# An attention and two-MLP kernel: where VectorE splits the weights, builds the keys of chunk 1 and takes the low part of x

## The chip, the cores and the metric

The program runs on one core of a Trainium2 chip. Its engines are TensorE (PE, with its weight loads as PEld), VectorE (DVE), ScalarE (ACT), GpSimd (POOL) and SyncE (SP), which issues most transfers. Each engine works through its own instructions in the order in which they are written and meets the others at semaphores. The metric is the device time of one execution in microseconds (us), lower is better.

## The reference

A linear attention with a decaying state over 4 sequences of 768 tokens and 8 heads of 48 features, and two MLPs (384 to 2048 to 384) over the 3072 tokens:

```python
for t in range(S):
    cur = np.einsum('bhd,bhe->bhde', u[None] * kt, vt)
    y[:, :, t] = np.einsum('bhd,bhde->bhe', rt, state + cur)
    state = w[None, :, :, None] * state + np.einsum('bhd,bhe->bhde', kt, vt)
...
h = x @ w_in                                        # first MLP
x = (np.maximum(h, 0) + alpha * np.minimum(h, 0)) @ w_out
h = x @ w_in2                                       # second MLP
out = (h * np.tanh(log(1 + exp(h)))) @ w_out2
```

## The kernel before

**Numbers.** Every matrix product of the MLPs is made of three products of split values: high part of the weights by high part of the data, low by high, high by low. So each weight block (128 hidden units of 16, a "slot": 768 columns) is read raw, copied to its high part on ACT (`split_hi`, L808) and subtracted to its low part (`split_lo`) on DVE (L684), or for the slots in `pool_slots` (0, 6, 10, 14 of the first MLP) on POOL (L461). Three raw buffers rotate: SP loads slot i when slot i - 3 has its low part.

**Attention.** The 3072 tokens are 24 chunks of 128; a chunk has two units v of two pairs of heads each. For a unit, keys (L315) and queries (L305) are scaled by powers of the decay, PE forms blocks of scores at seven levels (`score`, L1068, 104 small products), ACT writes the diagonal (`fill_diagonal`, L837) and copies the large blocks (`copy_high`, L849), DVE puts in the small ones with predicated copies, "the picks" (`pick_scores`, L601, 8 or 10 of them), and PE multiplies by the values and the state (`attend`, L1085 and L1091). `sum_state` (L1042) on PE and `advance_state` (L580) on DVE carry the state from chunk to chunk. When both units of a chunk are attended, ACT writes the high part of x (`x_hi_part`, L858 and L859), DVE the low part (`x_lo_part`, L617 and L619), and SP and ACT move rows of them between partitions (`fill_holes`, L325).

**Stages.** `first_tile` does attention alone, units 0 to 9 (chunks 0 to 4). PE scores unit v, in even v sums the state, multiplies the identity with itself (`warm`, L984, a result that nobody reads) and attends unit v - 1. DVE takes the picks of v and then scales keys (chunk c + 1) itself; POOL scales queries. `tile1` (t = 1 to 6) follows: 96 steps s, in each of which PE does `up(s)` (L1010, nine products of 128x512), then `down(s - 2)` (L1026, nine more), and between them in even steps `attend` of unit 8 + s/2 and `score` of unit 9 + s/2, in every fourth step (s = 3, 7, ...) `sum_state`. ACT takes both halves of the rectifier (L894, L895), DVE joins them (`activate`, L690), ACT writes the high part (`hi_part`, L814) and DVE the low part (`lo_part`, L674) of the result. `up(s)` waits for the low part of step s - 2, since two banks `hid` alternate. In even steps DVE then takes the picks of the unit scored in that step. In the tile t = 1 the splits of the first MLP's weights lie between: ACT in step j writes the high part of slot j + 4, DVE in step j the low part of slot j + 3. `tile2` is the second MLP, with no attention.

**The order around the change.** In the order on DVE all of it is written out by hand: activate, advance_state, x_lo_part, lo_part, picks, split_lo, sum_diagonal (L610). On ACT in an odd step: rectifier, hi_part, fill_diagonal of the coming unit, split_hi. On POOL two waits hold back work in chunk 5 until DVE's splits of slots 2 and 3 are done.

## Time and profile before

| | us |
|---|---|
| median of 3 runs | 991.45 |
| lowest and highest | 991.1, 991.75 |
| the profiled execution, its own time | 988.31 |
| its span, first to last instruction | 986.6 |
| busy in the span: PE, PEld | 964.5, 784.4 |
| DVE, ACT, POOL | 675.1, 618.9, 375.8 |

The profile has the program in 24025 instructions. PE is busy 98% of the span, and its granted clock has a mean of 0.992 of full speed (2.4 GHz). A time in a timeline is counted from the start of the span; "idle before <- X" names what ended an engine's idle time. The first matrix product of the first MLP starts at 62.97 us; before it lies the attention alone.

### The profile page before, as it was taken

To read this page: it belongs to the slowest core of one execution; us is meant where nothing else is said; L and a number is where in the kernel's file an instruction comes from. 1 tells how busy PE (TensorE), PEld (TensorE's weight loads), DVE (VectorE), ACT (ScalarE), POOL (GpSimd) and SP (SyncE) were. 2 spreads that over 40 slices of the span, in tenths; PEclk is the share of its full clock that TensorE was granted. 3 is DMA by queue.
4 is the path that set the end of the run, shared out by engine and by line. 5 is a ranking of instruction groups with operands and counts; after the bars stand their busy time and mean duration, and the time that the engine had idled before them with its cause. 6 is when DMAs were issued, how large, how long until landed. Compare 5 with 4: busy or idle time off the path is not lost.

```text
span 986.6 us, 24025 instructions
## 1 busy us (share of the span) xinstructions
PE 964.5 (98%) x9508; PEld 784.4 (80%) x9508; DVE 675.1 (68%) x1405; ACT 618.9 (63%) x1274; POOL 375.8 (38%) x664
## 2 busy tenths in 40 slices
PE   7889899999999999999999999999999999999997
PEld 4668678888888888888888888888888888888886
DVE  8997786666666666666653337877777777677775
ACT  6765545545554554455445658878777777787774
POOL 9989676667666676666501430000000000000000
PEclk8999899999999999999999999999999999999999
DMA  6353322111211131112004330000000000000000
GB/s 185 101 146 111 109 62 73 53 47 55 82 57 46 46 94 46 45 46 62 14 8 162 96 128 33 33 1 33 33 33 33 1 32 0 16 16 0 33 1 32
DMA packets 24617, 54.35 MB, mean 55 GB/s; under 512 B 4928, under 2 KB 12736, under 8 KB 24512
## 3 DMA queue, kind: packets, MB, share of 16 engines
q1 hardware_dynamic: 22688, 43.45, 14.8%
q10 hardware_dynamic: 1824, 9.47, 2.4%
q8 instruction: 70, 1.15, 0.5%
q14 instruction: 35, 0.29, 0.1%
HBM read 41.10 MB, written 9.44 MB: 51 GB/s over the span
## 4 chain that ended last, share of the span: by engine, by line
PE 89%; DVE 6%; ACT 2%; issue 1%; DMA 1%; SPq 0%; POOL 0%; DVEq 0%; ACTq 0%; POOLq 0%
PE acc L1026 40%; PE hid L1010 28%; PE lev L1010 10%; PE lev L1068 6%; DVE scores L601 3%; PE tok L1091 2%; PE tok L1085 2%; PE tok L1042 1%; DVE w_lo L684 1%; DVE hid L690 1%; DVE arena L315 1%; DMA neg_slope<-slope 1%; ACT scores L837 0%; PE hid L1068 0%; ACT w_hi L808 0%
## 5 line engine op out<-in xcount | busy, mean ns | idle before, releaser
L1010 PE MATMUL hid<-x_parts,w_hi 128*128 128x512 f32 x864 | 290.4, 390 | 0.6 <-DVE g_lo L674 0.6
L1026 PE MATMUL acc<-g_hi,w_hi 128*128 128x512 f32 x576 | 231.6, 402 | 0.0
L1026 PE MATMUL acc<-g_hi,w_lo 128*128 128x512 f32 x576 | 225.6, 392 | 0.0
L1010 PEld LDWEIGHTS hid<-x_parts,w_hi 128*128 128x128 f32 x864 | 162.6, 188 | 35.4 <-DVE g_lo L674 0.9
L601 DVE COPY_PREDICATED scores<-mask,lev 64x128 f32<-64x128 int8 x420 | 150.2, 358 | 29.9 <-ACT scores L849 18.1
L1010 PE MATMUL hid<-x_parts,w_lo 128*128 128x512 f32 x432 | 168.7, 390 | 0.0
L1026 PE MATMUL acc<-g_lo,w_hi 128*128 128x512 f32 x576 | 162.9, 391 | 0.0
L690 DVE SCALAR_TENSOR_TENSOR hid<-relu_neg,neg_slope,hid 128x512 f32<-128x512 f32 x96 | 72.5, 755 | 126.7 <-ACT hid L895 126.2
L894 ACT ACTIVATE relu_neg<-hid 128x512 f32<-128x512 f32 x96 | 57.3, 597 | 161.7 <-PE hid L1010 159.8
L1026 PEld LDWEIGHTS acc<-g_hi,w_hi 128*128 128x128 f32 x576 | 108.4, 188 | 23.9 <-issue 0.2
L1026 PEld LDWEIGHTS acc<-g_lo,w_hi 128*128 128x128 f32 x576 | 108.5, 188 | 23.2
L1026 PEld LDWEIGHTS acc<-g_hi,w_lo 128*128 128x128 f32 x576 | 108.6, 189 | 21.2
L305 POOL TENSOR_TENSOR arena<-arena,power 112x128 f32<-112x128 f32 x282 | 115.4, 444 | 2.1 <-DVE w_lo L684 2.1
L814 ACT ACTIVATE g_hi<-hid 128x512 fp32r<-128x512 f32 x96 | 57.5, 598 | 78.2 <-DVE hid L690 77.4
L455 POOL TENSOR_TENSOR arena<-arena,power_split 112x512 f32<-112x512 f32 x46 | 58.7, 1276 | 116.2 <-PE tok L1091 116.2
L737 DVE SCALAR_TENSOR_TENSOR arena<-arena 128x512 f32<-128x512 f32 x96 | 66.4, 692 | 51.7 <-ACT arena L934 51.7
L315 POOL TENSOR_TENSOR arena<-arena,power_rev 112x128 f32<-112x128 f32 x228 | 94.2, 448 | 19.2 <-PE lev L1068 17.6
L1010 PE MATMUL lev<-x_parts,w_hi 128*128 128x512 f32 x288 | 96.3, 389 | 0.0
L1010 PEld LDWEIGHTS hid<-x_parts,w_lo 128*128 128x128 f32 x432 | 81.4, 188 | 17.4 <-issue 0.2
L674 DVE TENSOR_TENSOR g_lo<-hid,g_hi 128x512 fp32r<-128x512 f32 x96 | 66.3, 691 | 39.5 <-ACT g_hi L814 39.3
L1068 PEld LDWEIGHTS lev<-arena 48*64 48x64 f32 x4472 | 74.3, 135 | 10.4 <-issue 10.4
L1068 PE MATMUL lev<-arena 48*64 48x32 f32 (+1 forms) x4472 | 79.1, 222 | 1.9 <-issue 1.2
(95 smaller groups left out, 1352.0 us busy)
## 6 DMA issues: line engine op xcount, KB each, us to landing
w_raw<-weights SPq DMA_DIRECT2D x32, 384.0 KB, 3.2
arena<-rkv SPq DMA_DIRECT2D x24, 384.0 KB, 3.2
arena<-rk_t SPq DMA_DIRECT2D x48, 192.0 KB, 3.4
arena<-rkv SPq DMA_DIRECT2D x24, 192.0 KB, 2.6
x_dram<-result ACTq DMA_DIRECT2D x6, 768.0 KB, 3.4
arena<-x_dram SPq DMA_DIRECT2D x6, 768.0 KB, 4.3
out<-result ACTq DMA_DIRECT2D x6, 768.0 KB, 3.3
x_parts<-y SPq DMA_DIRECT2D x142, 16.0 KB, 1.8
```

Of the source, the lines that this page charges most:

```text
L305: return engine.tensor_tensor(dst, src, spread(table[0:ROWS, pairs, 0:m], 2, CHUNK // (2 * m)), ALU.mult)
L315: return engine.tensor_tensor(dst, src, spread(table[0:ROWS, pairs, HALF - m:HALF], 2, CHUNK // (2 * m)), ALU.mult)
L455: nc.gpsimd.tensor_tensor(r_state[0:ROWS, x], spread(rk_rows[0:ROWS, par, 0, pairs], 1, 2), power_split[0:ROWS, :, pairs], ALU.mult).then_ ...
L601: nc.vector.copy_predicated(dst, pick, src).then_inc(pick_done if done < 2 * low_levels(rep) - 1 else mask_done, 1)
L674: nc.vector.tensor_tensor(g_lo[:, j % RING], hid[j % 2][:, 0:TILE], g_hi[:, j % RING].bitcast(F32), ALU.subtract).then_inc(glo_done, 1)
L690: nc.vector.scalar_tensor_tensor(hid[j % 2][:, 0:TILE], relu_neg[:, j % 2], neg_slope[:, j:j + 1], hid[j % 2][:, 0:TILE], ALU.mult, ALU.ad ...
L737: nc.vector.scalar_tensor_tensor(root[:, d], eps[:, d], 0.75, seed[:, d], ALU.add, ALU.mult).then_inc(root_done, 1)
L814: nc.scalar.activation(g_hi[:, j % RING], hid[j % 2][:, 0:TILE], ACT.Copy).then_inc(ghi_done, 1)
L894: nc.scalar.activation(relu_neg[:, j % 2], hid[j % 2][:, 0:TILE], ACT.Relu, scale=-1.0)
L1010: last = nc.tensor.matmul(to[:, 0:TILE], w[:, j, kt * P:(kt + 1) * P], x[:, par, kt], start=x is x_hi and w is w_hi and kt == 0, stop=x is ...
L1026: last = nc.tensor.matmul(acc[d][:, 0:TILE], w[:, j, cols], g[:, j % RING], start=j == 0 and g is g_hi and w is w_hi, stop=j == STEPS - 1 ...
L1068: last = nc.tensor.matmul(level_scores(banks, l)[tokens, 2 * q + u], k[rows, tokens], t[rows, wanted], start=True, stop=True)
```

## The change

It has five parts, none of which adds or removes work except three warm products on PE.

1. DVE in the tile t = 1: the splits of slots j + 3 are no longer done in each step behind the picks, but in step 0 (slot 3) and in odd steps (slots j + 3 and j + 4), where no picks are. sum_diagonal comes ahead of them.
2. ACT in the tile t = 1: in odd steps split_hi comes ahead of fill_diagonal, in even steps nothing changes.
3. DVE in the first stage: the keys of unit 2 (chunk 1) are scaled ahead of the first advance_state and picks; the low part of x for chunk 3 comes ahead of the picks of unit 8, not between the second and the third of them.
4. PE in the first stage: the warm products of unit 1 go (of 512 and of 256 columns); that of unit 9 and the last become three in a row.
5. PE: attend of unit 8 moves from the end of the first stage to step 0, behind up(0).

```diff
@@ attended_at
             v = FIRST - 2 + s // 2
-            return FIRST - 1 if s == 1 else v if s % 2 == 0 and FIRST <= v < UNITS else None
+            return FIRST - 2 + s if s < 2 else v if s % 2 == 0 and FIRST <= v < UNITS else None
@@ vector, first_tile
+                def keys_of(c, x):
+
+                    level = scale_half(c, x, False)
+                    for l in range(1, LEVELS):
+                        level(l)
...
+                    if v == 0:
+                        keys_of(1, 0)
                     if x == 0:
                         advance_state(c, token_bank(0, c))
                     if ends and x == 0:
-                        between = lambda n: x_lo_part(c - 1, 0, c - 1, token_bank(0, c - 1)) if n == 2 else None
-                    pick_scores(v, 0, between)
-                    if not ends:
-                        level = scale_half(c + 1, x, False)
-                        for l in range(1, LEVELS):
-                            level(l)
+                        x_lo_part(c - 1, 0, c - 1, token_bank(0, c - 1))
+                    pick_scores(v, 0)
+                    if not ends and v > 0:
+                        keys_of(c + 1, x)
@@ vector, tile1
                         pick_scores(unit, 1)
-                    if t == 1 and j < STEPS - EARLY and j + EARLY not in pool_slots:
-                        split_lo(j + EARLY)
                     if summing is not None and summing < CHUNKS - 1:
                         sum_diagonal(summing + 1, (summing + 1) % 2)
+                    if t == 1 and (j == 0 or j % 2):
+                        for i in range(j + EARLY, min(j + EARLY + 1 + j % 2, STEPS)):
+                            if i not in pool_slots:
+                                split_lo(i)
@@ scalar, tile1
                     hi_part(s, j)
+                    if unit is not None:
+                        copy_high(unit, 1)
+                    if t == 1 and j + EARLY + 1 < STEPS:
+                        split_hi(j + EARLY + 1)
                     if coming is not None:
                         fill_diagonal(coming)
-                    if unit is not None:
-                        copy_high(unit, 1)
                     if j == LAG1 - 1 and t > 1:
                         copy_out(t - 2, x2_dram[t - 2])
-                    if t == 1 and j + EARLY + 1 < STEPS:
-                        split_hi(j + EARLY + 1)
@@ tensor, first_tile
-                    for n in {0: (), 1: (PAIRS, PAIRS // 2)}.get(v, (PAIRS,)):
-                        warm(hid[1] if v == FIRST - 1 else acc[2], n)
-                    if v > 0:
+                    if PER_CHUNK <= v < FIRST - 1:
+                        warm(acc[2])
+                    if 0 < v < FIRST - 1:
                         attend(v - 1, 0)
-                warm(hid[1])
+                for _ in range(3):
+                    warm(hid[1])
```

How it moves instructions, at three places. First DVE in steps 2 to 4 of the tile t = 1 (g_lo is lo_part, scores the picks, w_lo a split, hid the activate). Before:

```order
L684 TENSOR_TENSOR w_lo<-w_raw,w_hi 128x768 [waits whi_done]
L690 SCALAR_TENSOR_TENSOR hid<-relu_neg,neg_slope,hid 128x512 [waits relu_done]
L576 MEMSET state 112x192 [waits av_done]
L674 TENSOR_TENSOR g_lo<-hid,g_hi 128x512 [waits ghi_done]
L610 TENSOR_REDUCE diag<-ruk 128x8 [waits fill_done,s_ruk]
L690 SCALAR_TENSOR_TENSOR hid<-relu_neg,neg_slope,hid 128x512 [waits relu_done]
```

The same stretch now, from the last of the picks of step 2 on:

```order
L601 COPY_PREDICATED scores<-mask,lev 64x4x2x16 [waits pick_done] x2
L692 SCALAR_TENSOR_TENSOR hid<-relu_neg,neg_slope,hid 128x512 [waits relu_done]
L576 MEMSET state 112x192 [waits av_done]
L676 TENSOR_TENSOR g_lo<-hid,g_hi 128x512 [waits ghi_done]
L608 TENSOR_REDUCE diag<-ruk 128x8 [waits fill_done,s_ruk]
L686 TENSOR_TENSOR w_lo<-w_raw,w_hi 128x768 [waits whi_done]
```

The split that stood between the picks of step 2 and activate of step 3 is gone from there, and one stands behind sum_diagonal of step 3.

Second, DVE at the start of the first stage, where the six rows of keys (arena<-arena,acc) of unit 2 move; a piece of the difference:

```order
-L601 COPY_PREDICATED scores<-mask,lev 64x4x8x4 [waits pick_done] x2
-L601 COPY_PREDICATED scores<-mask,lev 64x4x4x8 [waits pick_done] x2
-L315 TENSOR_TENSOR arena<-arena,acc 112x64x2 [waits score_done,rows_in1]
+L315 TENSOR_TENSOR arena<-arena,acc 112x64x2 [waits score_done,rows_in1,s_masks]
 L315 TENSOR_TENSOR arena<-arena,acc 112x32x4
 L315 TENSOR_TENSOR arena<-arena,acc 112x16x8
```

The keys stand now ahead of the first advance_state, and wait there for the scores of unit 0 and for the rows of chunk 1.

Third, PE between the scores of unit 9 (acc<-arena) and up(0) (hid<-x_parts). Before:

```order
L1068 MATMUL acc<-arena 64x32 x24
L984 MATMUL hid<-ident 128x512
L1085 MATMUL tok<-arena,state 48x128 x2
L1091 MATMUL tok<-scores,arena 48x128 x2
L1085 MATMUL tok<-arena,state 48x128 x2
L1091 MATMUL tok<-scores,arena 48x128 x2
L984 MATMUL hid<-ident 128x512
L1010 MATMUL hid<-x_parts,w_hi 128x512
```

Now:

```order
L1072 MATMUL acc<-arena 64x32 x24
L988 MATMUL hid<-ident 128x512 x3
L1014 MATMUL hid<-x_parts,w_hi 128x512
L1014 MATMUL hid<-x_parts,w_lo 128x512
L1014 MATMUL hid<-x_parts,w_hi 128x512
L1014 MATMUL hid<-x_parts,w_lo 128x512
L1014 MATMUL hid<-x_parts,w_hi 128x512
L1014 MATMUL hid<-x_parts,w_lo 128x512
```

attend of unit 8 (tok<-) no longer stands between the two warm products, but behind up(0).

## Rows read from the trace of the kernel before

**Rows 1.** Busy time by stretch: us, each engine's busy us, granted PE clock, DMA.

```profile
50.00:100.00 50.00, 46.56 (x751) 36.37 (x751) 40.70 (x91) 28.99 (x75) 46.05 (x76) 1.00 0.45 126
100.00:125.00 25.00, 21.86 (x298) 17.67 (x298) 19.27 (x42) 14.67 (x35) 15.34 (x27) 0.86 0.35 108
...
150.00:175.00 25.00, 25.00 (x338) 20.36 (x337) 16.63 (x39) 13.58 (x35) 17.05 (x35) 1.00 0.26 78
```

**Rows 2.** Waits of PE from 60 to 150 us: for whom, total us, times, longest.

```profile
PE tok L1091 <- DVE state L580: 2.2, 1, 2.2
...
PE tok L1042 <- DVE x_parts L619: 1.0, 1, 1.0
PE tok L1085 <- issue: 1.0, 1, 1.0
PE hid L1010 <- DVE g_lo L674: 0.6, 1, 0.6
```

**Rows 3.** The chain that ended last, behind the longest wait and later: start, us, what.

```profile
108.86 2.21 PE lev L1068 x86
111.07 4.14 PE acc L1026 x9
115.20 2.85 PE hid L1010 x9
...
122.15 0.57 PE tok L1091 x8
122.73 1.75 PE lev L1068 x94
124.48 2.28 PE acc L1026 x9
126.76 2.04 PE hid L1010 x9
```

**Rows 4.** Busy time in stretches of 2 us behind that wait, columns as in Rows 1.

```profile
110.00:112.00 2.00, 2.00 (x44) 1.76 (x37) 0.76 (x1) 1.18 (x3) 1.02 (x4) 0.50 0.09 28
...
116.00:118.00 2.00, 2.00 (x9) 1.59 (x8) 1.88 (x5) 0.00 (x0) 1.92 (x3) 0.81 0.00 0
```

**Rows 5.** Timeline of DVE in steps 3 to 5: start, us, instruction, idle before.

```profile
81.88 0.76 DVE L690 SCALAR_TENSOR_TENSOR hid<-relu_neg,neg_slope,hid 128x512 f32<-128x512 f32 x1
...
86.17 0.75 DVE L690 SCALAR_TENSOR_TENSOR hid<-relu_neg,neg_slope,hid 128x512 f32<-128x512 f32 x1 [1.72 <-ACT hid L895]
...
92.33 2.84 DVE L684 TENSOR_TENSOR w_lo<-w_raw,w_hi 128x768 fp32r<-128x768 f32 x1
95.20 0.76 DVE L690 SCALAR_TENSOR_TENSOR hid<-relu_neg,neg_slope,hid 128x512 f32<-128x512 f32 x1
```

**Rows 6.** All DVE splits from 60 to 150 us: shortest, median, longest in ns.

```profile
L684 DVE TENSOR_TENSOR w_lo<-w_raw,w_hi x12: 948/1040/3419, 62.1 to 143.6; 128x768 fp32r<-128x768 f32 x12
```

**Rows 7.** Timeline of DVE, first units, and last splits ahead of the MLP.

```profile
14.21 0.79 DVE L580 SCALAR_TENSOR_TENSOR state<-state,w_pow,tok 112x48 f32<-112x48 f32 x4 [1.02 <-PE tok L1042]
15.53 3.16 DVE L601 COPY_PREDICATED scores<-mask,lev 64x128 f32<-64x128 int8 x8 [0.54 <-ACT scores L849]
18.72 1.28 DVE L315 TENSOR_TENSOR arena<-arena,acc 112x128 f32<-112x128 f32 x6
...
25.98 3.17 DVE L601 COPY_PREDICATED scores<-mask,lev 64x128 f32<-64x128 int8 x8 [0.44 <-ACT scores L849]
...
62.06 1.82 DVE L684 TENSOR_TENSOR w_lo<-w_raw,w_hi 128x768 fp32r<-128x768 f32 x2
```

**Rows 8.** Timeline of ACT: the large blocks of unit 1.

```profile
18.16 1.78 ACT L849 ACTIVATE scores<-hid 64x256 f32<-64x256 f32 x7 [0.69 <-PE hid L1068]
```

**Rows 9.** Timeline of PE: scores of unit 1, and the warm products that go.

```profile
14.90 3.20 PE L1068 MATMUL hid<-arena 48*64 48x64 f32 x104 [0.82 <-POOL arena L305]
18.02 2.93 PE L984 MATMUL acc<-ident 128*128 128x512 f32 x4
```

**Rows 10.** Timeline of POOL: the keys of unit 10, beside which the moved splits fall.

```profile
59.42 2.41 POOL L315 TENSOR_TENSOR arena<-arena,power_rev 112x128 f32<-112x128 f32 x6
```

More of the change, by code:

```diff
@@ L646, in first_tile @@
                 sum_diagonal(0, 0)
[L647 to L649 removed]
+                keys_of(0, 1)
                 dve.wait_ge(s_masks, 2 * LOW + 2)
```

9 lines of the change are left out of this document (2 added, 7 removed).

## The prediction

> **What bounds the kernel now.** First the busy time by stretch [rows 1]. Between 150 and 175 us PE is busy for 25.00 of 25 us at the full clock, and from there to its last product it waits for nothing; from 50 to 100 us it is busy for 46.56 of 50 us, from 100 to 125 for 21.86 of 25, and there with a granted clock of 0.86. So whatever this change does, it does it before about 150 us, and every microsecond that PE loses there is one in the end time: nothing behind it has slack to give back. Second, who PE waits for in that part [rows 2]: 2.2 us once for DVE's state, 1.0 once for DVE's low part of x, 1.0 that is put down to "issue" and 0.6 once for DVE's low part g_lo. The third one has the same cause as the first as I read it: it is an attend (L1085, first of its group with a state), and advance_state on DVE ended just before it, late behind a split that took the 3.42 us that stand in [rows 6] as the longest. Third, the chain behind the 2.2 us wait [rows 3]: the products that follow it take 2.21, 4.14 and 2.85 us for groups that take 1.75, 2.28 and 2.04 us one turn later. The clock says why [rows 4]: 0.50 of 2.4 GHz, that is 1.2 GHz, from 110 us on, and in 116 to 118 it has come back for most of the time. PE had stood still for 2.2 us before the fall and was busy without a gap before the rise.
>
> Then DVE, whose lateness all this is [rows 5]. From activate of step 3 (81.88) to that of step 4 (86.17) are 4.29 us, in which DVE idles 1.72 for ACT: an odd step is set by ACT (high part, diagonal, split_hi, rectifier). From activate of step 4 to that of step 5 (95.20) are 9.03 us without a gap to speak of: activate, low part, ten picks and then the split, which alone takes 2.84. The split's own length is 0.95 us [rows 6]; it is longer where POOL works on the same stretch. Ahead of the MLP, DVE is busy without a gap from the picks of unit 2 (25.98 [rows 7]) to the picks of unit 9, and the first steps start when it is done.
>
> **The change, part by part.**
>
> *Splits out of the steps with picks.* Even steps with a split took DVE 92.33 - 86.17 = 6.16 us up to it [rows 5]; without it the next activate starts there. An odd step leaves DVE 4.29 us, of which activate and the low part take 2.0 (the low part ends 0.6 us after g_hi is ready) and sum_diagonal 0.5 in every second one. Two splits at 0.95 make 2.0 + 1.9 = 3.9, inside 4.29; where sum_diagonal stands (steps 3, 7, 11) only one split is left, since the other slot is POOL's: 2.0 + 0.5 + 0.95 = 3.45, with the 0.7 of advance_state beside ACT's high part. So a pair of steps on DVE falls to 6.16 + 4.29 = 10.45 us, against 9.03 + 4.29 = 13.3 in the worst pair before. PE needs for a pair two ups (2.04 each), two downs (2.28 and 2.04), scores (1.75) [rows 3] and an attend (eight products without a state take 0.57, so sixteen with one 1.1), 11.2 us, and 0.6 more where it sums a state. DVE is now ahead by 0.7 us or more per pair, where it fell back before. The three waits of 2.2, 1.0 and 1.0 us go: 4.2 us.
>
> *The clock.* With the 2.2 us of standstill gone, I take its consequence to go with it: (2.21 - 1.75) + (4.14 - 2.28) + (2.85 - 2.04) = 0.46 + 1.86 + 0.81 = 3.1 us [rows 3]. Ends: 0 if the clock falls all the same, 3.1 if it doesn't.
>
> *Price of the moved splits.* Each is exposed to POOL. The longest of the twelve, 3.42, is 2.5 us over its own 0.95 [rows 6]; in an odd step with 0.4 us of room that delays the next activate by up to 2.1 us. What would be late next is the picks of that step, and then the attend two steps later. Counting from up(s) at 0: the rectifier ends at 3.1, the picks at about 9.8, and the attend that needs them is due on PE at 11.2 + 2.0 = 13.2. 2.1 us late still fits, with 1.3 to spare; two such blocks in a row, less DVE's lead, would just touch. I take 0, the other end is 1 to 2 us.
>
> The Trainium skill, page "SBUF — State Buffer", section "Who interferes with whom", says that a DVE instruction with two SBUF inputs and a GpSimd instruction that reads SBUF exclude each other, the second one being blocked until the first is through. The trace agrees in kind: 0.948 us at best and 3.419 at worst for the same split [rows 6]. By it, two splits in a row could be held up twice in a step that had one; it speaks against this change, and would give the time of rival 2 below.
>
> *ACT's order.* split_hi ahead of fill_diagonal in odd steps: both lie ahead of the next rectifier in both orders, so nothing for the chain. It makes the high part of the second split's slot ready in time (one split_hi, 0.7 us, behind g_hi, while DVE still does its low part and the first split). The raw blocks come no later, since SP's loads hang on splits that are now earlier or as early. 0.
>
> *Keys of unit 2 ahead.* They cost 1.28 us [rows 7] wherever they stand. At their new place DVE idled 1.02 for PE's state sum and 0.54 for ACT's high blocks, 1.56 in all, so they hide there: the first picks stay at about 15.5. Gone behind them: 1.2 us. But the picks of unit 1 wait for ACT's blocks, which end at 18.16 + 1.78 = 19.94 [rows 8], and those for scores that POOL's queries and the low clock hold until 18.1 [rows 9]. They start at 20.1. Then 3.15 of picks, 1.2 of keys, 0.7 of state: the picks of unit 2 at 25.2, against 25.98 with its wait of 0.44 [rows 7]. So 0.8 us comes out of 1.6.
>
> *Warm products of unit 1.* 2.93 us at the low clock [rows 9] leave PE's queue; DVE is the bound there, so they give nothing by themselves except that the scores of unit 2 end before they are wanted (the 0.44 above). Scores at the low clock take 3.20 us [rows 9]: begun at 19.5 they end at 22.7, and ACT's blocks at 24.6, ahead of 25.2 even if the clock stays low till then. The scores of unit 3 then come some tenths late: up to 0.4 of the 0.8 may go.
>
> *Low part of x ahead of the picks of unit 8.* Same work, other order, on an engine without a gap: 0 for DVE. The rows that fill_holes moves are ready sooner, but on SP it stands behind the load of slot 3, which waits for POOL's split of slot 0; it has no row of its own here, and up(0) has 1.5 us of room for it (next point).
>
> *attend of unit 8 behind up(0), three warm products in a row.* PE no longer waits for the picks of unit 8. up(0) starts near 61.5 instead of 62.97, but up(2) needs the low part of step 0 on DVE, behind the picks of unit 9: PE will wait there as before (0.6 [rows 2]). The splits of slots 1 and 2 (62.06 [rows 7]) come at 61.3 and meet POOL's keys, which run to 59.42 + 2.41 = 61.8 [rows 10]: up to 0.5 of the 0.8 may be lost here. Both losses weighed, I carry 0.5 us to up(2); ends 0 and 0.8.
>
> *Sum.* 4.2 + 3.1 + 0.5 = 7.8 us. Against the profiled execution: 988.3 - 7.8 = 980.5, its span 986.6 - 7.8 = 978.8. The median of the timed runs lies 3.1 us over the profiled execution, which I carry unchanged: 991.45 - 7.8 = **983.7 us**. Own range of this case, with 0 to 0.8 in place of 0.5 and half a microsecond of spread of the runs: 982.8 to 984.7.
>
> **The rivals.**
>
> 1. *The clock falls all the same*, or falls at another place, since PE still waits before up(2) and its small products leave the array thinly used. For it: it fell at a time when no single wait was longer than 0.8 us, by the time of the 0.82 us gap of [rows 9], at whose end PE ran at half speed (3.20 us for scores that take 1.75 [rows 3]). Against: from 50 to 100 us it held at 1.00 with 3.4 us of gaps in it [rows 1]. Time: 991.45 - (4.2 + 0.5) = 986.8.
> 2. *POOL moves the stalls instead of removing them.* The blocks of 1 to 2.5 us fall now on pairs of splits. For it: the longest split, 3.42 us [rows 6]. Against: the room counted above. Time: one wait comes back as 1 to 2 us, with the clock full as after the other 1.0 us waits: 984.7 to 985.7; if the 2.2 us wait comes back with the clock behind it, and one of 1.0, only 7.8 - 6.3 = 1.5 is left: 990. The Trainium skill's rule above names the same mechanism.
> 3. *The change doesn't reach PE*, because DVE's lateness comes from ACT and PE themselves (an odd step is ACT's). Then only the start moves: 991. Against: 2.84 us of a split stand directly before the late activate [rows 5].
> 4. *Slower: the low clock stays in the attention-only stage.* The warm products of unit 1 were the dense work between 18 and 21 us, after which the clock was full. Without them PE goes on at 1.2 GHz with gaps. A unit then costs PE 3.2 (scores) + 2.0 (a warm product, two thirds of 2.93) + 1.5 + 0.6, 7.3 us, against some 5.2 on DVE (25.98 - 15.53 for two units [rows 7]): 2.1 us lost per unit. It eats the gain of 7.8 from the fourth such unit on, and over seven units gives 991.45 - 7.8 + 14.7 = 998. Against: at that clock PE has no gaps, the same state in which the clock rose in [rows 4].
>
> **How the numbers follow.** Forecast 0.68, clock all the same 0.12, POOL 0.09 (mostly the mild form), not reached 0.03, slower 0.05; 0.03 for more than forecast, should the 3.1 us between profile and timed runs contain a second fall of the clock that goes too (980.6). The range takes in the forecast, rival 1 and mild rival 2: 982.0 to 987.3. A measurement of this kernel tells 0.2% (2 us) from no change. Faster 0.91, same 0.04, slower 0.05.
>
> **What the profile of the changed kernel would show.** PE without a wait over 0.3 us from up(2) to its end; a granted clock of 1.00 from 100 to 125 us; DVE going from its last pick straight to activate in even steps of t = 1; splits in pairs behind the low part of odd steps, some of them over 1.5 us; the picks of unit 2 near 25.2, up(2) near 68.8. I am wrong if the clock stands at 0.5 anywhere between 25 and 150 us, if a split pair pushes an activate by more than 3 us, or if fill_holes holds up(0) beyond 63.5.

## The result, and the profile after

The changed kernel takes 993.24 us (median of 20 runs, 990.77 to 996.3), the kernel before beside it on the same chip 990.28 us (20 runs, 986.43 to 996.55). The ratio is 1.003, with a 95% interval of 1.0016 to 1.0044: slower by 0.3%. The forecast was 983.7 us with a range of 982.0 to 987.3, so it is wrong in size and in sign.

| | before | after |
|---|---|---|
| median of the timed runs, us | 990.28 | 993.24 |
| profiled execution, own time, us | 988.31 | 993.21 |
| its span, us | 986.6 | 991.4 |

The page of the profile after opens with the span, and with each engine's busy time, share and instructions. After that stands the group of the up products, whose idle time has a new owner:

```profile
span 991.4 us, 24020 instructions
...
PE 967.5 (98%) x9506; PEld 786.2 (79%) x9506; DVE 681.1 (69%) x1405; ACT 618.9 (62%) x1274; POOL 377.1 (38%) x664
...
L1014 PE MATMUL hid<-x_parts,w_hi 128*128 128x512 f32 x864 | 291.4, 392 | 7.2 <-DVE g_lo L676 5.4
```

The same stretches as in [rows 1], with the same columns, show where PE lost time: 41.08 busy us from 50 to 100 where there were 46.56. From 150 us on it is again busy without a gap.

```profile
50.00:100.00 50.00, 41.08 (x679) 30.87 (x672) 45.48 (x85) 25.07 (x69) 44.58 (x74) 0.98 0.47 130
100.00:125.00 25.00, 24.95 (x321) 19.99 (x322) 20.00 (x42) 15.63 (x35) 17.08 (x29) 0.90 0.36 110
150.00:175.00 25.00, 25.00 (x376) 20.21 (x376) 15.39 (x36) 13.99 (x36) 15.49 (x30) 1.00 0.16 45
```

PE's waits from 60 to 150 us (for whom, total us, times, longest) answer to [rows 2]. The waits of 2.2 us for the state and of 1.0 us for the low part of x, and the 1.0 us of "issue", are gone as forecast. One wait of 5.4 us for g_lo, DVE's low part, has come:

```profile
PE hid L1014 <- DVE g_lo L676: 5.4, 1, 5.4
PE hid L1014 <- DMA x_parts<-y: 1.8, 1, 1.8
PE acc L1072 <- issue: 0.5, 1, 0.5
PE tok L1089 <- issue: 0.4, 1, 0.4
```

Behind it, the chain that ended last (start, us, what) shows the split, activate, high part, low part and the up products:

```profile
85.92 11.73 DVE w_lo L686
97.65 0.68 DVE hid L692
98.35 0.61 ACT g_hi L818
98.98 0.70 DVE g_lo L676
99.72 4.21 PE hid L1014 x9
```

All splits of DVE from 60 to 150 us, in one row as in [rows 6] (shortest, median, longest in ns), with the new longest one:

```profile
L686 DVE TENSOR_TENSOR w_lo<-w_raw,w_hi x12: 947/1112/11810, 64.6 to 140.7; 128x768 fp32r<-128x768 f32 x12
```

DVE's timeline of step 3, which answers to [rows 5], gives the cause its name. The split of slot 7 stands behind sum_diagonal (L608), as the new order wants it. It takes 11.81 us, where the same instruction takes 0.95 at its shortest:

```profile
85.84 11.81 DVE L686 TENSOR_TENSOR w_lo<-w_raw,w_hi 128x768 fp32r<-128x768 f32 x1
97.57 0.74 DVE L692 SCALAR_TENSOR_TENSOR hid<-relu_neg,neg_slope,hid 128x512 f32<-128x512 f32 x1
```

POOL's timeline of the same stretch. L305 are the queries, L315 the keys, L482 the keys for the state, L461 POOL's own split, L455 the rows for the state, L468 and L472 the two products r*k and times the bonus:

```profile
84.67 2.43 POOL L305 TENSOR_TENSOR arena<-arena,power 112x128 f32<-112x128 f32 x6
87.05 1.01 POOL L482 TENSOR_TENSOR arena<-arena,power_tok 128x384 f32<-128x384 f32 x1
88.01 1.86 POOL L461 TENSOR_TENSOR w_lo<-w_raw,w_hi 128x768 fp32r<-128x768 f32 x1
89.81 1.30 POOL L455 TENSOR_TENSOR arena<-arena,power_split 112x512 f32<-112x512 f32 x1
91.07 2.45 POOL L315 TENSOR_TENSOR arena<-arena,power_rev 112x128 f32<-112x128 f32 x6
93.46 2.42 POOL L305 TENSOR_TENSOR arena<-arena,power 112x128 f32<-112x128 f32 x6
95.83 1.00 POOL L468 TENSOR_TENSOR ruk<-arena 128x384 f32<-128x384 f32 x1
96.91 1.59 POOL L472 TENSOR_TENSOR ruk<-ruk,bonus_tok 128x384 f32<-128x384 f32 x1
```

Each of these rows starts a few hundredths of a microsecond before the row ahead of it ends, until L472: it reads what L468 writes, and starts 0.08 us behind its end (95.83 + 1.00 = 96.83, then 96.91). DVE's split ends at 97.65, and L472, which started at that gap, takes 1.59 us instead of the 1.02 that it takes undisturbed. So DVE asked at 85.84, was kept out while POOL went on, without a break, through 19 operations (the fourth of the queries, begun 0.04 us before that moment, the last two of them, then one, one, one, six, six and L468), and got in at the first gap, 11 us later. Activate of step 4 then starts at 97.57, where it could have started near 87.6 (it starts 1.8 us behind the start of this split in run 3 below, where nothing holds the split up). PE runs dry for 5.42 us, and its clock falls. The nine products behind the wait take 4.21 us where nine of their kind take 2.04 [rows 3]. All engines' busy time in stretches of 2 us behind the wait, columns as in [rows 1], has the granted clock at 0.50, which is 1.2 GHz, and back at full some 5 us after PE has begun again:

```profile
100.00:102.00 2.00, 2.00 (x5) 1.54 (x6) 1.88 (x5) 1.60 (x3) 0.00 (x0) 0.50 0.06 22
106.00:108.00 2.00, 2.00 (x78) 1.83 (x71) 2.00 (x2) 2.00 (x7) 1.43 (x3) 1.00 0.04 8
```

To see how much that is worth I set the traces of all kernels beside each other by one mark: the start of ACT's high part g_hi of a step of t = 1. Before, step 0 has it at 67.93 us, step 3 at 82.67, step 4 at 86.95, step 16 at 159.84, and step 88 at 556.94. After minus before:

| mark | step 0 | step 3 | step 4 | step 16 | step 88 |
|---|---|---|---|---|---|
| changed kernel | +2.53 | +1.47 | +11.39 | +4.50 | +4.85 |

The spans differ by 991.4 - 986.6 = 4.8 us, the last column. The table takes them apart: 2.5 us later out of the first stage, 1.1 us won in steps 0 to 3, 9.9 lost in one step, 6.9 won back from there to step 16 (where the old kernel had its own three stalls and its low clock), and 0.35 afterwards. Without the first stage the change cost 4.50 - 2.53 = 1.97 us up to step 16, where -7.3 was forecast. Both remainders were to be explained: some 9 us in the tile t = 1, and 2.5 of the first stage. The distance from step 0 to step 16 repeats well: in the three traces with the old place of the splits and no waits added (before, runs 2 and 4) it agrees within 0.06 us. The mark of step 0 itself does not, as will be seen.

### The profile page after: what moved, and what is told of

Same layout as the page of the kernel before. It is cut to its first block, busy times and chain, and to the rows that moved or that the text cites. A ratio compares the mean times of both kernels' runs of the same rounds, so it can differ in the third digit from the quotient of the medians.

```text
span 991.4 us, 24020 instructions
## 1 busy us (share of the span) xinstructions
PE 967.5 (98%) x9506; PEld 786.2 (79%) x9506; DVE 681.1 (69%) x1405; ACT 618.9 (62%) x1274; POOL 377.1 (38%) x664
## 3 DMA queue, kind: packets, MB, share of 16 engines
q8 instruction: 70, 1.15, 0.5%
## 4 chain that ended last, share of the span: by engine, by line
PE 92%; DVE 5%; ACT 1%; issue 1%; DVEq 0%; ACTq 0%
PE acc L1030 40%; PE hid L1014 29%; PE lev L1014 10%; PE lev L1072 7%; DVE scores L601 2%; PE tok L1095 2%; PE tok L1089 2%; DVE w_lo L686 1%; PE tok L1046 1%; PE acc L988 1%; DVE arena L315 0%; PE hid L1072 0%; DVE hid L692 0%; ACT g_hi L818 0%; DVE state L580 0%
## 5 line engine op out<-in xcount | busy, mean ns | idle before, releaser
L305 POOL TENSOR_TENSOR arena<-arena,power 112x128 f32<-112x128 f32 x282 | 115.7, 444 | 2.1 <-DVE w_lo L686 2.1
L455 POOL TENSOR_TENSOR arena<-arena,power_split 112x512 f32<-112x512 f32 x46 | 58.7, 1275 | 119.2 <-PE tok L1095 117.3
L315 POOL TENSOR_TENSOR arena<-arena,power_rev 112x128 f32<-112x128 f32 x228 | 95.0, 452 | 19.3 <-PE lev L1072 17.8
```

The costliest lines, as they stand in the source:

```text
L305: return engine.tensor_tensor(dst, src, spread(table[0:ROWS, pairs, 0:m], 2, CHUNK // (2 * m)), ALU.mult)
L315: return engine.tensor_tensor(dst, src, spread(table[0:ROWS, pairs, HALF - m:HALF], 2, CHUNK // (2 * m)), ALU.mult)
L455: nc.gpsimd.tensor_tensor(r_state[0:ROWS, x], spread(rk_rows[0:ROWS, par, 0, pairs], 1, 2), power_split[0:ROWS, :, pairs], ALU.mult).then_ ...
```

## The experiments

The theories, by the order in which they came up. **Lock-out** (A): DVE's split can't get in while POOL runs without a break; if POOL breaks its run, the forecast gain appears. **Warm products** (B): the first stage loses because PE's dense work of unit 1 is gone and its clock stays low longer; parts 4 and 5 of the change then cost about what stands at step 0. **Chance** (C): when the clock falls in the first stage varies from one execution to the next, whatever the kernel. And, for the gain itself, **place** against **lock-out before**: does the kernel before lose its 7 us because a split stands ahead of activate, or because that split, too, was kept out by POOL?

"Before" and "changed" in the edits name the kernel that a diff starts from; a line of three dots stands for lines left out. Line numbers differ by a few from kernel to kernel.

**1. The splits and ACT's order alone (parts 1 and 2), on the kernel before.**

```diff
-                    if t == 1 and j < STEPS - EARLY and j + EARLY not in pool_slots:
-                        split_lo(j + EARLY)
...
+                    if t == 1 and (j == 0 or j % 2):
+                        for i in range(j + EARLY, min(j + EARLY + 1 + j % 2, STEPS)):
+                            if i not in pool_slots:
+                                split_lo(i)
...
```

The lines left out are ACT's, as in the change.

> The kernel before with parts 1 and 2 of the change alone (splits in odd steps, split_hi ahead of fill_diagonal). Theory A (the time is lost where a split of DVE is shut out by GpSimd's unbroken run of operations: 11.81 us for one split in the changed kernel, with a wait of 5.4 us on PE behind it and a low clock behind that): about as slow as the changed kernel or slower by what the rest of it brings, 992 to 995 against 990, with one split of 5 us or more in step 3 and a wait of PE for g_lo. Theory B (the time is lost in the attention-only stage, where the clock is low from 20 to 29 us and again from 37 to 40 without the warm products): faster than before by 3 us or more, since the stage is the old one and the waits of 2.2, 1.0 and 1.0 us go.

Measured: 993.3 us (989.68 to 996.28), before 990.51, ratio 1.0012 (0.9994 to 1.003). The trace has the same lock-out in the same step, of the same length, in DVE's timeline:

```profile
86.45 11.89 DVE L684 TENSOR_TENSOR w_lo<-w_raw,w_hi 128x768 fp32r<-128x768 f32 x1
```

From step 0 to step 16 this kernel loses 1.78 us against before, the changed one 1.97. So parts 1 and 2 alone make the loss, and it recurs: two executions of two kernels, 11.81 and 11.89 us, with a wait of PE for g_lo of 5.4 us in the one and 6.3 in the other. The time itself can't be told from no change, since the interval includes 1. With the first stage as before, step 0 was nevertheless late by 3.23 us. That speaks for chance (C), for this kernel's PE has all its warm products.

**2. The splits and ACT's order put back, the rest of the change kept.** The diff is that of run 1, with + and - exchanged, on the changed kernel.

> The changed kernel with parts 1 and 2 undone (splits behind the picks again, fill_diagonal ahead of split_hi); parts 3 to 5 stay. Theory A: the long split goes, and the time is that of the kernel before or better, 988 to 990.5. Theory B: the low clock stays in the first stage and up(2) starts some 1 to 3 us later than before: 991 to 994. Both can hold, then about 991.5 with splits no longer than 3.5 us.

Measured: 989.83 us (987.35 to 998.54), before 990.51, ratio 0.999 (0.9967 to 1.0014): no difference. From step 0 to step 16 it is -0.06 us against before, with the two long stalls of before in the list of PE's waits:

```profile
PE tok L1093 <- DVE state L580: 2.2, 1, 2.2
PE tok L1087 <- issue: 1.0, 1, 1.0
```

What parts 3 to 5 give or take is thus too small for this run: its interval leaves room from 3.3 us less to 1.4 us more, so it can't judge the 0.5 us of the forecast.

**3. POOL waits for DVE's splits: the changed kernel, with breaks in POOL's run.** POOL waits in chunks 5 to 8, ahead of the keys for the state and ahead of the second half's queries, until DVE has made the split that would otherwise meet its run. There are six such waits, for the splits of slots 5, 7, 9, 11, 13 and 15; the expectations say five, which is a miscount. Nothing else is changed.

```diff
...
+                if before_state is not None:
+                    lo_split_reached(pool, before_state)
                 scale_for_state(c, par, uses)
...
+                if before_queries is not None:
+                    lo_split_reached(pool, before_queries)
                 queries_of(c, par, 1)
...
-            chunk(5, 1, 3)
-            chunk(6, 0, 4, slots=(6,))
-            chunk(7, 1, 4, slots=(10,))
-            chunk(8, 0, 5, slots=(14,))
+            chunk(5, 1, 3, before_queries=5)
+            chunk(6, 0, 4, slots=(6,), before_state=7, before_queries=9)
+            chunk(7, 1, 4, slots=(10,), before_state=11, before_queries=13)
+            chunk(8, 0, 5, slots=(14,), before_state=15)
```

> The changed kernel with five more waits on GpSimd, which stands still until the splits of DVE in steps 1, 3, 5, 7, 9 and 11 are done (ahead of scale_for_state and of the queries of the second unit in chunks 5 to 8), as two such waits in chunk 5 do already. Theory A: no split longer than about 2 us, no wait of PE over 1 us between up(2) and the end, clock full from 75 us on; time 4 to 9 us under the changed kernel, 984 to 989. Theory B: 1 to 2 us under it at most. If GpSimd itself becomes late by its waits, PE waits for keys or queries (L305, L315) and the time rises.

Measured: 985.52 us (982.37 to 986.26), before 990.51, ratio 0.9931 (0.9905 to 0.9957). The split of step 3 is short, and PE's stretches are nearly full at the full clock. DVE's row, then the stretches from 50 to 125 us, columns as in [rows 1]:

```profile
83.23 1.20 DVE L690 TENSOR_TENSOR w_lo<-w_raw,w_hi 128x768 fp32r<-128x768 f32 x1
```

```profile
50.00:100.00 50.00, 46.62 (x750) 36.35 (x751) 43.02 (x100) 31.29 (x79) 41.27 (x71) 1.00 0.44 127
100.00:125.00 25.00, 25.00 (x338) 20.06 (x337) 18.51 (x43) 15.13 (x34) 18.11 (x32) 1.00 0.36 111
```

From step 0 to step 16: -6.57 us, against the -7.3 of the forecast and the +1.97 of the changed kernel. This is the run that shows the lock-out as the cause: 8.5 us come back by waits alone (7.7 between the medians of the two kernels), though the waits can only make POOL later.

**4. PE's part alone (parts 4 and 5), on the kernel before.**

```diff
...
-                    for n in {0: (), 1: (PAIRS, PAIRS // 2)}.get(v, (PAIRS,)):
-                        warm(hid[1] if v == FIRST - 1 else acc[2], n)
-                    if v > 0:
+                    if PER_CHUNK <= v < FIRST - 1:
+                        warm(acc[2])
+                    if 0 < v < FIRST - 1:
                         attend(v - 1, 0)
-                warm(hid[1])
+                for _ in range(3):
+                    warm(hid[1])
```

The lines left out are those of `attended_at`, as in the change.

> The kernel before with parts 4 and 5 alone (no warm products behind the scores of unit 1, three in a row behind those of unit 9, attend of unit 8 behind up(0)). Theory B: low clock beyond 21 us in the first stage, PE late for DVE there, 1 to 3 us over before: 991 to 993.5. Theory A: within 1 us of before, 989.5 to 991.

Measured: 992.56 us (987.37 to 996.49), before 990.51, ratio 1.0008 (0.9985 to 1.003): not told from no change. Step 0 is 3.07 us late in its trace and nothing is lost from there to step 16. That fits B and C alike, since run 1, which keeps the warm products, was 3.23 us late as well.

**5. One of the six waits: only the one ahead of the keys for the state in chunk 6.**

```diff
...
-            chunk(6, 0, 4, slots=(6,))
+            chunk(6, 0, 4, slots=(6,), before_state=7)
```

> The changed kernel with one more wait on GpSimd: in chunk 6, ahead of scale_for_state, until the split of slot 7 (DVE, step 3) is done. If the whole loss comes from the one split of 11.8 us: that split takes under 2.2 us, the wait of 5.4 us on PE goes, the clock stays full, and the time is within 1.5 us of the kernel with five such waits, 985 to 987, against 993.2 for the changed kernel. If the splits behind it (1.84, 1.16, 1.72 us) matter too, one of them grows over 3 us and PE waits 1 to 2 us again: 987 to 990.

Measured: 985.14 us (982.51 to 987.65), before 990.25, ratio 0.9938 (0.9917 to 0.9959). From step 0 to step 16 it wins 5.4 us, so one wait brings 7.4 of the 8.5 us. One wait of 0.6 us of PE for the picks (scores) is left, behind a later pair of splits that no wait covers (2.57 and 1.75 us).

The row for POOL's queries beside the split tells something about the mechanism that was not expected. It gives shortest, median and longest of the six operations in ns. First the changed kernel, then this one:

```profile
L305 POOL TENSOR_TENSOR arena<-arena,power x6: 410/466/468, 84.7 to 86.6; 112x128 f32<-112x128 f32 x6
```

```profile
L305 POOL TENSOR_TENSOR arena<-arena,power x6: 403/452/1165, 85.4 to 88.1; 112x128 f32<-112x128 f32 x6
```

DVE's split was ready in the one 1.17 us behind the first of these six (85.84 against 84.67), in the other 1.16 us behind it (86.56 against 85.40): at the same place. Yet in the one it was kept out for 11 us, and in the other one of POOL's six operations gave way (1165 ns instead of some 450), before POOL had come to the added wait. Runs 1, 3 and 6 fit in: refused at 1.09 us without a wait, admitted at 0.78 and 1.15 with one. So in these five traces the added wait decides it and not the alignment of the two engines, but it acts from ahead, by some operations, and why it does is not shown by any row. No run puts a wait there that is long met, so whether the wait must still be open is not shown either.

**6. A wait of POOL for its own results, in place of a wait for DVE.** Such a wait lets nothing else be late: its semaphore is set by POOL's instruction just ahead.

```diff
...
+                if own_wait:
+                    pool.wait_ge(q_done[0], c + 1)
                 scale_for_state(c, par, uses)
+                if own_wait:
+                    pool.wait_ge(kstate_done, c + 1)
...
-            chunk(6, 0, 4, slots=(6,))
+            chunk(6, 0, 4, slots=(6,), own_wait=True)
```

> The changed kernel in which GpSimd does not wait for DVE, but twice in chunk 6 for an operation of its own: ahead of scale_for_state for its queries, behind it for that operation. Theory A1 (DVE gets in at any gap in GpSimd's run that comes of a wait for its own result, as at the end of the 11.81 us, between L468 and L472): the split of step 3 ends within 3.5 us, the rest as with one wait for DVE, 985 to 987.5. Theory A2 (a gap of 0.1 us is not enough or DVE got in there by chance; it takes a GpSimd that stands still for DVE): the split takes 10 us or more again, 992 to 994.

Measured: 984.61 us (982.06 to 986.76), before 990.25, ratio 0.9926 (0.9898 to 0.9954). The split takes 1.27 us and the queries beside it are stretched as in run 5 (DVE's row, and POOL's):

```profile
86.36 1.27 DVE L690 TENSOR_TENSOR w_lo<-w_raw,w_hi 128x768 fp32r<-128x768 f32 x1
```

```profile
85.21 3.14 POOL L305 TENSOR_TENSOR arena<-arena,power 112x128 f32<-112x128 f32 x6
88.43 1.01 POOL L482 TENSOR_TENSOR arena<-arena,power_tok 128x384 f32<-128x384 f32 x1
```

A gap of 0.08 us at each of the two waits (85.21 + 3.14 = 88.35, then 88.43) is all that POOL pays, and they remove the lock-out like the wait for DVE. The split was again let in ahead of the wait, 2 us before that gap, so it is not the gap itself that admits it here. A pair of splits that the two waits don't cover stands at 2.84 and 1.75 us, and PE waits 1.3 us for the picks behind it; up to step 16 it wins 4.7 us.

**7. The six waits, with the first stage of before:** run 1 and run 3 together, without parts 3 to 5.

> The kernel before with parts 1 and 2 of the change and the five waits on GpSimd; the attention-only stage is the old one (parts 3 to 5 left out). If parts 3 to 5 gain what the prediction carried (0.5 us): 0 to 1 us over the kernel with all parts and the five waits, 985.5 to 986.5. If the removed warm products cost time (theory B): 1 to 3 us under it, 982.5 to 984.5.

Measured: 985.42 us (982.11 to 986.99), before 990.25, ratio 0.993 (0.9902 to 0.9958). From step 0 to 16 it is -6.65 us. The longest split is 1.56 us. Step 0 comes at 70.33 us, 2.41 late, in spite of the first stage of before: against B, as in run 1. The time lies 0.1 us under the 985.5 to 986.5 that was named for a gain of 0.5 us by parts 3 to 5, and above B's 982.5 to 984.5.

**8. The six waits, the changed order, and the warm products of unit 1 back.** The diff is on run 3.

```diff
-                    if PER_CHUNK <= v < FIRST - 1:
-                        warm(acc[2])
+                    for n in {0: (), 1: (PAIRS, PAIRS // 2), FIRST - 1: ()}.get(v, (PAIRS,)):
+                        warm(acc[2], n)
```

> The changed kernel with the five waits on GpSimd and the warm products of unit 1 (512 and 256 columns) put back, all else as in the change. Theory B: the clock is back at full by 22 us in most executions, 1 to 2 us under the kernel with the five waits, 983.5 to 984.5. If the low clock of the first stage is a matter of when the clock falls and not of these products: no difference beyond 1 us, 984.5 to 986.5.

Measured: 982.88 us (981.57 to 985.14), before 990.25, ratio 0.9919 (0.9892 to 0.9946). Step 0 comes at 68.31 us and step 16 at 153.13, -7.1 us between them. It beats the kernel before by 0.8%.

**9. The kernel before, with waits of POOL for its own results behind every group of chunks 5 to 8.** No split is moved. If the split's place was the cause of the stalls of before, they stay; if it was that a split in that place was kept out, they go.

```diff
...
+                def own(semaphore, count):
+                    if gaps:
+                        pool.wait_ge(semaphore, count)
...
                 keys_of(c, par, 0)
+                own(key_done, 2 * c + 1)
...
                 queries_of(c, par, 0)
+                own(q_done[0], c + 1)
                 scale_for_state(c, par, uses)
+                own(kstate_done, c + 1)
                 for i in slots:
                     split_lo(i)
+                    own(wlo_pool, sum(k <= i for k in pool_slots))
                 rows_for_state(c, par, 0)
+                own(rstate_done, 2 * c - 1)
...
                 keys_of(c, par, 1)
+                own(key_done, 2 * c + 2)
                 queries_of(c, par, 1)
+                own(q_done[1], c + 1)
```

> The kernel before, in which GpSimd waits for its own last result behind every group of operations in chunks 5 to 8 (keys, queries, state rows, splits), so that DVE can get in between; the splits stay behind the picks, nothing else is changed. Theory P (the place of the splits is the cure): the splits fall to 1 to 1.5 us, but a pair of steps on DVE still takes 11.4 us or more against 11.2 to 11.8 on PE, and waits of 1 us and more stay: 987 to 989. Theory L (the lock-out is the whole trouble, the place hardly matters): no wait of PE over 0.7 us behind up(2), clock full from there: 983 to 986.

Measured: 985.98 us (984.37 to 989.84), before 990.87, ratio 0.9954 (0.9937 to 0.9971). The answer lies between the two. The split that stood at 92.33 in [rows 5] with 2.84 us takes 0.96 here, and PE's wait of 2.2 us for the state is gone, but from 66 to 150 us PE still waits three times:

```profile
PE tok L1102 <- issue: 1.5, 1, 1.5
PE tok L1096 <- issue: 1.3, 1, 1.3
PE hid L1021 <- DVE g_lo L685: 1.0, 1, 1.0
```

From step 0 to step 16 it wins 2.9 us, where the moved splits with the same waits win 6.7 (next run). So of the kernel before's 7 us at least some 3 was lock-out, and at most some 4 hangs on the place of the splits. The waits did not take all delay away: one split still takes 2.64 us, beside POOL's own split, a single operation of 1.84 us with no place for a wait in it (DVE's row, and POOL's), and PE's wait of 1.3 us stands behind it:

```profile
129.69 2.64 DVE L695 TENSOR_TENSOR w_lo<-w_raw,w_hi 128x768 fp32r<-128x768 f32 x1
```

```profile
129.67 1.84 POOL L461 TENSOR_TENSOR w_lo<-w_raw,w_hi 128x768 fp32r<-128x768 f32 x1
```

The wait of 1.5 us follows a split that took its bare 0.96; that one is the place's. The median, 4.9 us better than before, would put more of the gain on the lock-out; the profile is one execution, and the medians of two sets of runs differ by chance too.

**10. The changed kernel, with the waits of run 9 and the warm products of run 8.**

> The changed kernel with the same waits of GpSimd for its own results in chunks 5 to 8 and with the warm products of unit 1 put back; no wait for DVE is added. If gaps alone are as good as waits for DVE everywhere: within 1 us of the kernel with five waits for DVE and the warm products, 982 to 984.5. If a pair of splits is now and then shut out by the parts between the gaps (six operations of 0.42 us): one split of 2 to 3 us, 984.5 to 986.

Measured: 982.71 us (981.56 to 987.27), before 990.87, ratio 0.9937 (0.9915 to 0.9959). From step 0 to step 16: -6.7 us. The longest split is 1.72 us. Waits for POOL's own results do what waits for DVE do.

**11 and 12. Runs 3 and 8 once more, in one session.** The kernels are those of runs 3 and 8, to tell the worth of the warm products from chance.

> The changed kernel with five waits of GpSimd for DVE once more, beside the one with the warm products of unit 1: 984.5 to 986 by both theories; the difference to the next one is the question.

> The same with the warm products of unit 1 put back, once more. Theory B (these products pay): 1.5 to 3 us under the one without, as in the single comparison so far. Theory C (that comparison was chance of when the clock falls in the first stage): within 1 us of it.

Measured: run 11 983.58 us (981.38 to 991.24), before 990.87, ratio 0.9943 (0.9923 to 0.9963); run 12 982.66 us (981.59 to 984.59), ratio 0.9924 (0.9902 to 0.9947). Between the medians of the two lie 0.9 us, inside the 1 us of theory C; run 11 came out under its 984.5 to 986. Taken together with their first runs: without the warm products of unit 1 a mean of 984.45 us with a standard error of 0.60 (18 runs); with them 983.24 with one of 0.35 (19 runs, run 10 among them, which has other waits). The difference is 1.2 us with a standard error of 0.7: suggestive and no more, since a 95% interval of it includes 0.

The marks of all kernels, minus those of before:

| | step 0 | step 3 | step 4 | step 16 | step 0 to 16 |
|---|---|---|---|---|---|
| changed kernel | +2.53 | +1.47 | +11.39 | +4.50 | +1.97 |
| 1 splits alone | +3.23 | +2.08 | +12.08 | +5.01 | +1.78 |
| 2 splits back | +1.42 | +1.42 | +1.42 | +1.36 | -0.06 |
| 3 six waits | -0.07 | -1.14 | -1.14 | -6.64 | -6.57 |
| 4 PE's part alone | +3.07 | +3.06 | +3.06 | +3.08 | +0.01 |
| 5 one wait | +3.25 | +2.19 | +2.19 | -2.17 | -5.4 |
| 6 own result, chunk 6 | +3.06 | +1.98 | +1.99 | -1.66 | -4.7 |
| 7 old first stage, six waits | +2.41 | +1.25 | +1.25 | -4.24 | -6.65 |
| 8 six waits, warm | +0.39 | -0.76 | -0.76 | -6.71 | -7.1 |
| 9 before, own results | +2.16 | +2.36 | +2.36 | -0.75 | -2.9 |
| 10 own results, warm | -0.04 | -1.19 | -1.19 | -6.77 | -6.7 |
| 11 as 3 | +1.99 | +0.82 | +0.82 | -5.22 | -7.2 |
| 12 as 8 | +0.50 | -0.64 | -0.63 | -6.64 | -7.1 |

The first column answers what the first stage does. With the first stage of before, step 0 has its mark at 67.93, 71.15, 70.33 and 70.08 us (before, runs 1, 7 and 9), on average 69.9. With that of the change it stands at 70.45, 69.34, 67.85, 71.17, 70.98 and 69.91 (the changed kernel, runs 2, 3, 5, 6 and 11), on average 69.95. The profile of before was the early end of a spread of 3 us, not its middle. A third group was left with both: the changed order with the warm products of unit 1 kept (runs 8, 10 and 12) has the mark at 68.31, 67.89 and 68.43, on average 68.2. Of the eleven other traces only those of before and of run 3 are as early.

## Why the prediction was wrong

**The step that failed** is "Price of the moved splits", where it says "I take 0, the other end is 1 to 2 us". The bound came from the longest split in the trace, 3.42 us [rows 6], as if the longest delay seen were the longest that could come. What limits the delay is how long POOL runs without a gap behind the moment at which DVE asks, and that stood in the trace of before. From 80 to 100 us POOL was busy for 19.92 us of 20; the stretch of the profile before, columns as in [rows 1]:

```profile
80.00:100.00 20.00, 20.00 (x302) 16.19 (x300) 14.54 (x25) 10.69 (x25) 19.92 (x33) 1.00 0.37 106
```

The 2.84 us of the split in [rows 5] was short only because DVE came late to it. It asked at 92.33, and POOL's next gap lay between L468 and L472:

```profile
93.34 1.01 POOL L468 TENSOR_TENSOR ruk<-arena 128x384 f32<-128x384 f32 x1
94.44 1.60 POOL L472 TENSOR_TENSOR ruk<-ruk,bonus_tok 128x384 f32<-128x384 f32 x1
```

The change moved the request to the start of that run of POOL, and so lengthened the delay from 1.9 to 10.9 us. With that read, the upper end of the delay would have been some 11 us, and the room counted (1.3 us) would have said that PE runs dry. What the runs showed in place of the 0: the split of step 3 took 11.81 us, PE stood for 5.42 us with a low clock behind it, and the tile came out 1.97 us longer up to step 16 instead of 7.3 shorter. The rule of the Trainium skill, page "SBUF — State Buffer", section "Who interferes with whom", that the second of two such instructions is blocked until the first is through, was weighed with the same fault: what matters here is that "the first" was followed at once by the next, until 19 had gone by. The page's rule agrees with the traces where a split takes 1.07 to 1.2 us and in run 9, where one takes 2.64 beside an operation of 1.84, and falls short of those of 11.81 and 11.89.

**The three waits and the clock, 4.2 + 3.1 = 7.3 us**, were right as a size, once run 3's waits are added, and not for the change as it was made. With the lock-out gone, steps 0 to 16 win 6.57, 7.2, 6.65, 7.1, 6.7 and 7.1 us (runs 3, 11, 7, 8, 10, 12), 6.9 on average. The place of the splits as the cause was right in part, by 4 us at most: run 9, which moves no split, wins 2.9 of it. So that a split stood directly before the late activate, as the prediction holds against rival 3, was not the whole reason for the old stalls.

**The start, 0.5 us**, was not won by the change as made: the averages of the step 0 mark are 69.9 and 69.95 us. What the forecast gave for it hung on the trace of one execution, and between executions of the same kernel this mark moves by 2 us (runs 3 and 11: 67.85 and 69.91). Two signs in it missed. The picks of unit 2 came at 26.60 and not at 25.2. The keys of unit 2 do not hide in DVE's idle time, as "Keys of unit 2 ahead" has it: at their new place they wait 1.64 us for PE's scores of unit 0, and the first picks begin behind them and the state at 16.96, and not at 15.5. DVE's timeline after has both, the last row being the one that answers to that at 25.98 in [rows 7]:

```profile
15.07 1.27 DVE L315 TENSOR_TENSOR arena<-arena,acc 112x128 f32<-112x128 f32 x6 [1.64 <-PE lev L1072]
...
16.96 3.14 DVE L601 COPY_PREDICATED scores<-mask,lev 64x128 f32<-64x128 int8 x8
...
26.60 3.16 DVE L601 COPY_PREDICATED scores<-mask,lev 64x128 f32<-64x128 int8 x8 [0.16 <-ACT scores L853]
```

And up(0) waited 1.8 us for fill_holes' rows, until 66.1, past the 63.5 that was named as a limit. That has a price: PE is busy without a gap from there through up(2), which no longer waits for DVE as in [rows 2]. It starts at 72.67, while the low part of step 0 was ready at 71.09 + 0.69 = 71.78, so the rows cost some 0.9 us here (PE's rows of up(0) and up(2), then DVE's low part):

```profile
66.12 0.47 PE L1014 MATMUL hid<-x_parts,w_hi 128*128 128x512 f32 x1 [1.75 <-DMA x_parts<-y]
...
72.67 0.50 PE L1014 MATMUL hid<-x_parts,w_hi 128*128 128x512 f32 x1
```

```profile
71.09 0.69 DVE L676 TENSOR_TENSOR g_lo<-hid,g_hi 128x512 fp32r<-128x512 f32 x1 [0.67 <-ACT g_hi L818]
```

By the start of up(2), where the prediction wanted its 0.5 us, the changed first stage stands at 72.0 us on average over its six traces, the old one at 71.3 over its four: later by 0.8, within their spread of 3 us.

**The median of before** was 991.45 in the three runs ahead of the prediction and 990.3 to 990.9 in those beside the experiments. That is 0.6 to 1.2 us of any miss of the absolute time, and it doesn't bear on the sign.

**The rivals.** Rival 2, POOL moves the stalls, named the right mechanism, and the page of the Trainium skill beside it spoke of that mechanism, but the size was wrong: 984.7 to 985.7 us mild, 990 at worst, and 0.09 of the chance. Its worst form was bounded by the stalls of before coming back, not by a new one of 5.4 us with the low clock behind it. Rival 4, the low clock in the attention-only stage, did show in part. Granted clock in stretches of the first stage, PE alone (sum, busy us, clock, DMA); first the changed kernel, then run 1, then run 8, both of which have the warm products of unit 1:

```profile
20.00:26.00 6.00, 5.75 (x129) 0.50 0.51 134
26.00:32.00 6.00, 6.00 (x118) 0.69 0.16 44
```

```profile
20.00:26.00 6.00, 6.00 (x129) 0.50 0.43 111
26.00:32.00 6.00, 6.00 (x123) 0.62 0.15 38
```

```profile
20.00:26.00 6.00, 4.32 (x132) 1.00 0.41 119
```

Run 1 shows that the clock can stand at 0.50 from 20 to 26 us with these products too. But over all fourteen traces, one of each kernel or repeat, the two groups differ in that stretch: the clock is 0.50 in all seven that lack them (the changed kernel and runs 2 to 6 and 11), and of the seven that have them 0.50 in two (runs 1 and 7) and 0.78 to 1.00 in five (before 0.90, run 8 1.00, run 9 0.78, run 10 0.89, run 12 0.87). So taking them out is a likely part of why the start won nothing: the prediction gave it 0 to 0.4 us. Its worth in time is the 1.2 us, standard error 0.7, of runs 3, 8, 10, 11 and 12, and stays open. A loss of the rival's size (2.1 us a unit, for seven units) is in no trace of a kernel without these products.

**What stays open** is why some of DVE's requests get in at a plain boundary between two operations of POOL (splits of 1.07 to 1.2 us), others at none of the 18 that POOL passed in the changed kernel, and how a wait on POOL that lies still ahead lets one in. A finer record of the two engines' requests would be wanted; no run here tells it. Open is also why runs 8, 10 and 12 start early, whether by chance or by the warm products in the changed order.

**The version that comes of it** is the changed order, with POOL's run broken by waits and the warm products of unit 1 kept: 982.7 to 982.9 us in three kernels (runs 8, 10 and 12), against 990.25 to 990.87 before, with ratios of 0.9919 (0.9892 to 0.9946), 0.9937 (0.9915 to 0.9959) and 0.9924 (0.9902 to 0.9947). That is 0.6 to 0.8%, near the 0.8% which was forecast, but for a kernel with waits on POOL that the change did not have and without one of its parts.

## What to carry to other kernels

Bound the delay of a moved VectorE operation by the unbroken run of GpSimd that it would now meet, read from GpSimd's timeline at the new moment, and not by the longest such operation that the old trace happens to hold. Where a steady stream of GpSimd work lies beside short VectorE operations that PE hangs on, put a wait into it, if only for its own last result: here two such waits cost 0.08 us each and gave back 6.7 us by the marks up to step 16, 8.6 between the medians of run 6 and the changed kernel. And set the start-up stage of two single profiles beside each other only when you know how far it moves between executions of one kernel.

## What was not expected of the hardware

- One operation of VectorE with two SBUF inputs, 0.95 us long, was held up for 10.9 us while GpSimd ran 19 operations back to back (11.81 and 11.89 us in two kernels). It got in at the first gap in GpSimd's work, of 0.08 us.
- With a wait added behind the operations that GpSimd was at, the VectorE operation got in ahead of the wait itself: at the same offset of 1.16 to 1.17 us into the same six operations it was refused in the changed kernel and admitted in run 5.
- The first fall of TensorE's clock comes at different times in executions of one kernel: from 14 to 20 us the granted clock was 0.54 in run 3 and 0.97 in run 11, which are the same kernel, and 0.50 from 20 to 26 us in both. Their marks of step 0 stand at 67.9 and 69.9 us.
- Between 429 and 440 us PE stops in 7 of the 14 traces for 0.6 to 1.1 us, amid a unit's scores or right behind them, with no releaser in the records. From step 16 to step 88 these kernels come out 0.9 to 2.9 us longer than before does, the most in run 7, whose clock is at 0.81 from 431 to 440 us. It is not in before, nor in the changed kernel, nor in runs 1, 5, 6, 10 and 11, and so is a part of the spread of the runs. In run 8's timeline of PE:

```profile
427.18 1.82 PE L1076 MATMUL lev<-arena 48*64 48x64 f32 x101
...
429.85 0.30 PE L1076 MATMUL lev<-arena 48*64 48x32 f32 x3 [0.85 <-issue]
```
